# Second mixture: block products and output tiles alternate three times a pair of slices in place of eight

## The chip, the cores and the metric

The kernel runs on one core of a Trainium2 chip. The metric is the device time of one execution in microseconds (us), the median of several runs; lower is better. Five engines work side by side, each through its own list of instructions in order: TensorE (PE: matmuls; its weight loads are a row of their own, PEld), VectorE (DVE), ScalarE (ACT), GpSimd (POOL), and SyncE (SP), which issues transfers here. They wait for each other through semaphores only.

## What is computed

A gated attention over 768 steps and 16 heads gives 1536 tokens of width 384. A gated feed-forward layer (width 1536) follows, and then the second mixture: four experts of width 1024, all applied to every token and weighted. The change touches only this last part.

```python
def _moe2_ref(x, domain_probs, w1, w2) -> np.ndarray:
    N, D = x.shape                                    # 1536, 384
    E = w1.shape[0]                                   # 4
    p = domain_probs / (domain_probs.sum(-1, keepdims=True) + 1e-09)
    out = np.zeros((N, D), dtype=np.float32)
    for e in range(E):
        h = np.maximum(x @ w1[e], 0.0)                # (1536, 1024)
        out += p[:, e:e + 1] * (h @ w2[e])
    return out.astype(np.float32)
```

## The kernel before

Every matrix product is made in float32 out of three matmuls on rounded parts: high by high, high by low, low by high.

The second mixture goes through 16 pairs of slices. A pair is 256 of the 1024 hidden units of one expert. For a pair the hidden values are a 2 by 3 arrangement of blocks, two slices of 128 units by three groups of 512 tokens; each block fills one of six PSUM banks, A to F. Pair 0 is made plainly (`hidden_plain`: 54 matmuls of 512 columns in a row). Pairs 1 to 15 use a scheme with fewer multiplications: 15 **block products**, numbered 0 to 14, of sums of weight blocks with sums of token blocks. Each product is three matmuls of 512 columns (L1706 to L1708) into one bank; some banks take several products in turn. Between these, ScalarE copies a bank's state out (`keep`, L999) and VectorE adds or subtracts a kept copy to or from another bank (`combine`, L1375), so that each bank ends as a hidden block. ScalarE then applies the relu and rounds (`round_hidden`, L970: the high part), and VectorE makes the low part (`split_bank`, L1312). Only then is the bank free for the next pair.

An **output tile** is 128 tokens by 384 outputs of the previous pair's hidden values times the second weights: six matmuls of 384 columns (L1453 to L1455) into one of two small banks, out_ps0 for even tiles and out_ps1 for odd ones. There are 12 a pair, 0 to 11. VectorE adds a finished tile to the result in SBUF (`add_up`, L1329; L1326 for pair 0). TensorE may start tile n only when `add_up` of tile n - 2, which sat in the same small bank, is done (semaphore s_acc).

What sets the order is written out by hand. On TensorE it is `sums_and_outputs(pair)`: the 15 products of `pair`, with tiles of `pair - 1` between, of which the last (from `LAG` = 9 on) come in the next call, as tiles of `last - 1`. The loops over pairs on ScalarE and on VectorE are written to match. A number's place in `MULS` is its place among the products, from which the waits are worked out; `COPIES` and `ADDS` do the same for copies and combinations. For the last pair VectorE's list has an order of its own (`if pair == NPAIR - 1`). In pair 1 the rounded parts of the token sums are still being made: `split_sum` (L1318) on VectorE stands ahead of the loop, with `add_up(0, 0)` to `add_up(0, 2)` between.

After the last pair's products TensorE does what is left of pair 14's tiles and then pair 15's 12 tiles, and SyncE sends each result tile off when it is accumulated.

## Time and profile before

| | us |
|---|---|
| runs | 690.18, 690.23, 692.04 |
| median | 690.23 |
| span of the profiled execution | 689.6 |
| of it, hidden_plain and pairs 1 to 15's products and tiles, on TensorE | about 316 to 686.7 |
| one pair of slices, from a place to the same place a pair later | 23.0 |

The profiled execution's span, from its first to its last instruction, is 0.6 us under the median. No longer time of the same execution is given, so the 0.6 us stands for what lies around the span.

In the profile an engine's busy time is the sum of its instructions. TensorE's matmuls overlap each other in the records, so the distance between the starts of two matmuls tells what one costs, not its recorded length. In a timeline a row gives the start, the length, the engine, the line of the kernel, the operation, and written tile <- read tiles; a bracket at its end says how long the engine had been idle and who ended that.

### The profile page before, as it was taken

Reading aid. Unit: us, or ns where it says so; the run is one execution under the profiler, and the core shown is the slowest. Engines: PE = TensorE matmul, PEld = TensorE weight load, DVE = VectorE, ACT = ScalarE, POOL = GpSimd, SP = SyncE. Lnnn points to the kernel's source line nnn. Section 1 sums busy time; section 2 is a strip of 40 time slices with the busy share of each in tenths; the row PEclk is TensorE's granted clock in tenths of the full one; section 3 lists DMA queues with packets and bytes.
Section 4 is the critical chain, followed back from the end, with each engine's and each line's share of the span. In section 5 each row is a group of like instructions: output and inputs, shape, how many; then the busy total and the mean of one; then the engine's idle time right before and its main releaser. Section 6 shows DMA issues by size and latency. Waiting matters only on the chain.

```text
span 689.6 us, 10745 instructions
## 1 busy us (share of the span) xinstructions
PE 680.8 (99%) x3987; PEld 632.7 (92%) x3987; DVE 461.4 (67%) x820; ACT 266.4 (39%) x485; POOL 327.2 (47%) x416
## 2 busy tenths in 40 slices
PE   8999999999999999999999999999999999999998
PEld 7788999999999999998999999999999999999997
DVE  6875747555565544118978867886787678767876
ACT  4524533223522252227534333433343334343430
POOL 3569561111111116773394567456745674577200
PEclk9999999999999999999999999999999999999999
DMA  9896490009102001000011110111011101100003
GB/s 154 163 217 173 106 139 1 10 2 118 20 5 74 1 1 47 1 5 19 1 47 46 47 47 0 47 47 46 1 47 48 46 1 47 46 24 1 23 1 138
DMA packets 72230, 34.56 MB, mean 50 GB/s; under 512 B 53872, under 2 KB 71664, under 8 KB 72176
## 3 DMA queue, kind: packets, MB, share of 16 engines
q1 hardware_dynamic: 71728, 33.85, 22.8%
q8 instruction: 32, 0.52, 0.4%
q14 instruction: 22, 0.18, 0.1%
q10 hardware_dynamic: 448, 0.00, 0.0%
HBM read 30.89 MB, written 2.36 MB: 48 GB/s over the span
## 4 chain that ended last, share of the span: by engine, by line
PE 92%; SPq 3%; DVE 1%; POOL 1%; DMA 1%; issue 1%; ACT 0%; POOLq 0%
PE out_ps L1453 13%; PE out_ps L1454 13%; PE out_ps L1455 13%; PE hid_ps L1446 7%; PE hid_ps L1448 7%; PE hid_ps L1447 6%; PE at_ps L1708 5%; PE at_ps L1707 5%; PE at_ps L1706 4%; PE hid_ps L1707 2%; PE hid_ps L1708 2%; PE hid_ps L1706 2%; SPq L488 2%; PE at_ps L1531 2%; PE at_ps L1545 1%; PE at_ps L1585 1%
## 5 line engine op out<-in xcount | busy, mean ns | idle before, releaser
L1329 DVE SCALAR_TENSOR_TENSOR x<-out_ps,prob,x 128x384 f32<-128x384 f32 x180 | 110.3, 613 | 57.8 <-PE out_ps L1455 57.8
L1454 PE MATMUL out_ps<-early_r,late_r 128*128 128x384 f32 x384 | 129.4, 337 | 0.0
L1455 PE MATMUL out_ps<-early_r,late_r 128*128 128x384 f32 x384 | 129.3, 337 | 0.0
L1453 PE MATMUL out_ps<-early_r,late_r 128*128 128x384 f32 x384 | 129.0, 336 | 0.0
L722 POOL TENSOR_TENSOR hid_lo<-act_sb,hid_hi 128x384 fp32r<-128x384 f32 x44 | 44.8, 1019 | 159.6 <-ACT hid_hi L949 159.6
L999 ACT COPY late<-at_ps 128x512 f32<-128x512 f32 x105 | 61.8, 588 | 101.8 <-PE at_ps L1708 98.7
L1295 DVE TENSOR_TENSOR act_sb<-hid_ps,act_sb 128x384 f32<-128x384 f32 x48 | 26.0, 541 | 79.1 <-PE hid_ps L1448 79.1
L1453 PEld LDWEIGHTS out_ps<-early_r,late_r 128*128 128x128 f32 x384 | 72.1, 188 | 6.1 <-DVE x L1329 0.2
L1454 PEld LDWEIGHTS out_ps<-early_r,late_r 128*128 128x128 f32 x384 | 72.0, 188 | 5.6
L1455 PEld LDWEIGHTS out_ps<-early_r,late_r 128*128 128x128 f32 x384 | 72.1, 188 | 0.0
L949 ACT CAST hid_hi<-act_sb 128x384 fp32r<-128x384 f32 x48 | 24.6, 512 | 83.9 <-DVE act_sb L1295 83.9
L738 POOL TENSOR_TENSOR early<-stage 128x128 f32<-128x128 f32 x15 | 7.0, 467 | 102.4 <-PE at_ps L1708 102.4
L1708 PE MATMUL at_ps<-late_r,early_r 128*128 128x512 f32 x135 | 53.6, 397 | 0.0
L1375 DVE TENSOR_TENSOR at_ps<-at_ps,late 128x512 f32<-128x512 f32 x75 | 52.1, 695 | 0.5
L1706 PE MATMUL at_ps<-late_r,early_r 128*128 128x512 f32 x135 | 52.4, 388 | 0.0
L1446 PE MATMUL hid_ps<-xn_hi,wvh 128*128 128x384 f32 x141 | 49.2, 349 | 0.9 <-POOL wvl L652 0.9
L775 POOL TENSOR_TENSOR early_r<-early,early_r 128x1408 fp32r<-128x1408 f32 x15 | 48.5, 3236 | 0.0
L1707 PE MATMUL at_ps<-late_r,early_r 128*128 128x512 f32 x120 | 47.3, 394 | 0.0
L1448 PE MATMUL hid_ps<-xn_hi,wvl 128*128 128x384 f32 x141 | 47.3, 335 | 0.0
L1447 PE MATMUL hid_ps<-xn_lo,wvh 128*128 128x384 f32 x141 | 47.2, 335 | 0.0
L1453 PE MATMUL out_ps<-hid_hi,woh 128*128 128x384 f32 x132 | 46.3, 350 | 0.0
L1446 PE MATMUL hid_ps<-xn_hi,wgh 128*128 128x384 f32 x132 | 45.2, 342 | 0.2 <-DVE act_sb L1282 0.2
(301 smaller groups left out, 1617.4 us busy)
## 6 DMA issues: line engine op xcount, KB each, us to landing
stage<-in_moe_w_dram SPq DMA_DIRECT2D x32, 384.0 KB, 3.6
stage<-in_moe_w_out_dram SPq DMA_DIRECT2D x4, 576.0 KB, 5.4
out_dram<-x SPq DMA_DIRECT2D x12, 192.0 KB, 1.9
stage<-in_moe_w_gate_dram SPq DMA_DIRECT2D x8, 216.0 KB, 4.1
stage<-in_moe_w_val_dram SPq DMA_DIRECT2D x8, 216.0 KB, 4.2
a_tm<-in_alpha_dram SPq DMA_DIRECT2D x9, 192.0 KB, 4.5
k_tm<-in_k_dram SPq DMA_DIRECT2D x9, 192.0 KB, 5.4
q_tm<-in_q_dram SPq DMA_DIRECT2D x9, 192.0 KB, 5.3
```

Source lines behind the costliest of these rows:

```text
L999: act.copy(tcp[n], bank).then_inc(s_copy, 1)
L1329: dve.scalar_tensor_tensor(out=a, in0=part, scalar=p, in1=a, op0=ALU.mult, op1=ALU.add).then_inc(s_acc, 1)
L1375: dve.tensor_tensor(bank, bank, tcp[part], op).then_inc(s_add, 1)
L1446: pe.matmul(dst, ah, bh, start=(n == 0), stop=False)
L1447: pe.matmul(dst, ah, bl, start=False, stop=False)
L1448: mm = pe.matmul(dst, al, bh, start=False, stop=(n == last))
L1453: pe.matmul(dst, ah, bh, start=first, stop=False)
L1454: pe.matmul(dst, ah, bl, start=False, stop=False)
L1455: return pe.matmul(dst, al, bh, start=False, stop=last)
L1706: pe.matmul(bank, ah, bh, start=first, stop=False, skip_group_check=True)
L1707: pe.matmul(bank, ah, bl, start=False, stop=False, skip_group_check=True)
L1708: pe.matmul(bank, al, bh, start=False, stop=True, skip_group_check=True).then_inc(s_mul, 1)
```

## The change

TensorE's order is changed, and the two other engines' orders with it. No instruction is added or removed: the counts of products, tiles, copies and combinations stay the same.

- On TensorE a pair's products and tiles now form three groups each: products 8, 6, 10, then tiles 8 to 11 of the pair before last and tile 0 of the last; products 7, 0, 13, 12, then tiles 1 to 3; products 14, 4, 1, 11, then tiles 4 to 7; products 2, 9, 3, 5, which run on into the next pair's 8, 6, 10. `LAG` goes from 9 to 8. Products 11 and 1 change places.
- On ScalarE the copy after product 14 goes behind the rounding of bank F.
- On VectorE the `add_up` calls are spread differently. In the stretch ahead of the loop `add_up(0, 1)` and `add_up(0, 2)` are taken out from between the `split_sum` calls. The last pair no longer has an order of its own.

```diff
-        MULS = (8, 6, 10, 7, 0, 13, 12, 14, 4, 11, 1, 2, 9, 3, 5)
+        MULS = (8, 6, 10, 7, 0, 13, 12, 14, 4, 1, 11, 2, 9, 3, 5)
-        LAG = 9
+        LAG = 8
...
-                act.wait_ge(s_mul, nth(MULS, q, 14))
-                keep(4, bank_a)
                 if pair > 1:
                     act.wait_ge(s_tile, NTILE * (pair - 1))
                 act.wait_ge(s_add, nth(ADDS, q, 9))
                 round_hidden(bank_f, pair, 1, 2)
+                act.wait_ge(s_mul, nth(MULS, q, 14))
+                keep(4, bank_a)
...
             split_sum(4)
-            add_up(0, 1)
             split_sum(1)
             split_sum(2)
-            add_up(0, 2)
             split_sum(9)
...
                 combine(bank_f, 1, ALU.subtract)
-                add_up(pair - 1, 3)
+                add_up(pair - 1, 1)
                 dve.wait_ge(s_add, nth(ADDS, q, 7))
                 dve.wait_ge(s_copy, nth(COPIES, q, 2))
                 combine(bank_f, 2, ALU.subtract)
-                add_up(pair - 1, 4)
+                add_up(pair - 1, 2)
+                add_up(pair - 1, 3)
+                split_bank("F", 1, 2)
                 dve.wait_ge(s_mul, nth(MULS, q, 4))
                 dve.wait_ge(s_copy, nth(COPIES, q, 4))
                 combine(bank_d, 4, ALU.subtract)
-                split_bank("F", 1, 2)
                 dve.wait_ge(s_mul, nth(MULS, q, 11))
                 dve.wait_ge(s_copy, nth(COPIES, q, 8))
                 combine(bank_a, 8, ALU.subtract)
-                add_up(pair - 1, 5)
                 dve.wait_ge(s_mul, nth(MULS, q, 10))
                 dve.wait_ge(s_copy, nth(COPIES, q, 7))
                 combine(bank_e, 7, ALU.subtract)
+                add_up(pair - 1, 4)
+                add_up(pair - 1, 5)
+                split_bank("A", 1, 0)
                 add_up(pair - 1, 6)
-                split_bank("A", 1, 0)
                 add_up(pair - 1, 7)
...
                 split_bank("E", 0, 0)
-                add_up(pair - 1, 8)
-                split_bank("C", 0, 2)
                 dve.wait_ge(s_mul, nth(MULS, q, 5))
                 dve.wait_ge(s_copy, nth(COPIES, q, 5))
                 combine(bank_b, 6, ALU.subtract)
-                if pair == NPAIR - 1:
-                    add_up(pair - 1, 9)
+                split_bank("C", 0, 2)
                 dve.wait_ge(s_add, nth(ADDS, q, 8))
                 combine(bank_d, 5, ALU.add)
-                if pair < NPAIR - 1:
-                    add_up(pair - 1, 9)
-                add_up(pair - 1, 10)
+                add_up(pair - 1, 8)
                 dve.wait_ge(s_add, nth(ADDS, q, 1))
                 dve.wait_ge(s_copy, nth(COPIES, q, 9))
                 combine(bank_b, 9, ALU.subtract)
-                if pair == NPAIR - 1:
-                    add_up(pair - 1, 11)
+                add_up(pair - 1, 9)
                 split_bank("D", 1, 1)
-                if pair < NPAIR - 1:
-                    add_up(pair - 1, 11)
-                else:
-                    add_up(pair, 0)
+                add_up(pair - 1, 10)
                 split_bank("B", 0, 1)
-                if pair < NPAIR - 1:
-                    add_up(pair, 0)
-                add_up(pair, 1)
-                add_up(pair, 2)
-            for t in range(3, NTILE):
+                add_up(pair - 1, 11)
+                add_up(pair, 0)
+            for t in range(1, NTILE):
                 add_up(NPAIR - 1, t)
```

On TensorE the whole new order is in one place, and reads:

```diff
                 bank_free("A")
                 mul(bank_a, 8, True)
-                if q:
-                    out_tile(last - 1, 9)
-                    out_tile(last - 1, 10)
                 bank_free("F")
                 mul(bank_f, 6, True)
-                if q:
-                    out_tile(last - 1, 11)
-                out_tile(last, 0)
                 bank_free("E")
                 mul(bank_e, 10, True)
+                if q:
+                    for t in range(LAG, NTILE):
+                        out_tile(last - 1, t)
+                out_tile(last, 0)
                 kept(0)
                 mul(bank_a, 7)
                 bank_free("C")
                 mul(bank_c, 0, True)
-                out_tile(last, 1)
-                out_tile(last, 2)
                 kept(8)
                 mul(bank_f, 13)
                 bank_free("B")
                 mul(bank_b, 12, True)
-                out_tile(last, 3)
+                for t in range(1, 4):
+                    out_tile(last, t)
                 kept(2)
                 mul(bank_a, 14)
-                out_tile(last, 4)
                 bank_free("D")
                 mul(bank_d, 4, True)
+                kept(1)
+                mul(bank_b, 1)
                 kept(4)
                 mul(bank_a, 11)
-                out_tile(last, 5)
-                out_tile(last, 6)
-                kept(1)
-                mul(bank_b, 1)
-                out_tile(last, 7)
+                for t in range(4, LAG):
+                    out_tile(last, t)
                 kept(7)
                 mul(bank_d, 2)
                 kept(6)
                 mul(bank_c, 9)
                 kept(9)
                 mul(bank_e, 3)
-                out_tile(last, 8)
                 kept(3)
                 mul(bank_b, 5)
```

The order of the built programs shows it at three places. First TensorE where one pair passes into the next: products 5 (at_ps1), 8 (at_ps0) and then, before, tile 9 of the pair before last:

```order
L1706 MATMUL at_ps1<-late_r,early_r 128x512
L1707 MATMUL at_ps1<-late_r,early_r 128x512
L1708 MATMUL at_ps1<-late_r,early_r 128x512
L1706 MATMUL at_ps0<-late_r,early_r 128x512
L1707 MATMUL at_ps0<-late_r,early_r 128x512
L1708 MATMUL at_ps0<-late_r,early_r 128x512
L1453 MATMUL out_ps1<-early_r,late_r 128x384
L1454 MATMUL out_ps1<-early_r,late_r 128x384
L1455 MATMUL out_ps1<-early_r,late_r 128x384
```

TensorE at the same place after the change (its lines are numbered 11 lower): products 5, 8, then 6 (out_ps2) and 10 (hid_ps1), before any tile:

```order
L1695 MATMUL at_ps1<-late_r,early_r 128x512
L1696 MATMUL at_ps1<-late_r,early_r 128x512
L1697 MATMUL at_ps1<-late_r,early_r 128x512
L1695 MATMUL at_ps0<-late_r,early_r 128x512
L1696 MATMUL at_ps0<-late_r,early_r 128x512
L1697 MATMUL at_ps0<-late_r,early_r 128x512
L1695 MATMUL out_ps2<-late_r,early_r 128x512
L1696 MATMUL out_ps2<-late_r,early_r 128x512
L1697 MATMUL out_ps2<-late_r,early_r 128x512
L1695 MATMUL hid_ps1<-late_r,early_r 128x512
L1696 MATMUL hid_ps1<-late_r,early_r 128x512
L1697 MATMUL hid_ps1<-late_r,early_r 128x512
```

The tiles that stood between products 8, 6 and 10 now follow product 10 in one run of five.

Second, VectorE ahead of its loop and at the start of pair 1, before. L1326 is `add_up` of pair 0 (tiles 0, 1, 2, 3 in order), L1318 `split_sum`, L1312 the last block of pair 0, L1375 the first combination:

```order
L1326 TENSOR_SCALAR x2<-out_ps0,prob 128x384
L1318 TENSOR_TENSOR v_last<-early,late_r 128x512
L1312 SCALAR_TENSOR_TENSOR late_r<-hid_ps0,late_r 128x512
L1318 TENSOR_TENSOR late_r<-early,late_r 128x512
L1326 TENSOR_SCALAR x2<-out_ps1,prob 128x384
L1318 TENSOR_TENSOR late_r<-v_late,late_r 128x512
L1318 TENSOR_TENSOR late_r<-early,late_r 128x512
L1326 TENSOR_SCALAR x2<-out_ps0,prob 128x384
L1318 TENSOR_TENSOR late_r<-v_late,late_r 128x512
L1318 TENSOR_TENSOR late_r<-early,late_r 128x512 x2
L1375 TENSOR_TENSOR out_ps2<-out_ps2,late 128x512
L1326 TENSOR_SCALAR x2<-out_ps1,prob 128x384
```

VectorE at the same place after the change:

```order
L1326 TENSOR_SCALAR x2<-out_ps0,prob 128x384
L1318 TENSOR_TENSOR v_last<-early,late_r 128x512
L1312 SCALAR_TENSOR_TENSOR late_r<-hid_ps0,late_r 128x512
L1318 TENSOR_TENSOR late_r<-early,late_r 128x512
L1318 TENSOR_TENSOR late_r<-v_late,late_r 128x512
L1318 TENSOR_TENSOR late_r<-early,late_r 128x512
L1318 TENSOR_TENSOR late_r<-v_late,late_r 128x512
L1318 TENSOR_TENSOR late_r<-early,late_r 128x512 x2
L1373 TENSOR_TENSOR out_ps2<-out_ps2,late 128x512
L1326 TENSOR_SCALAR x2<-out_ps1,prob 128x384
L1373 TENSOR_TENSOR out_ps2<-out_ps2,late 128x512
L1326 TENSOR_SCALAR x2<-out_ps0,prob 128x384
```

Between `add_up` of tile 0 and of tile 1 stand eight 512-wide instructions and the first combination, where three stood.

Third, VectorE in the last pair, before, from the two combinations of bank C (at_ps2) on; L1312 are the splits of E, C, D and B, and L1329 the tiles 8, 9, 10, 11:

```order
L1375 TENSOR_TENSOR at_ps2<-at_ps2,late 128x512 x2
L1312 SCALAR_TENSOR_TENSOR late_r<-hid_ps1,late_r 128x512
L1329 SCALAR_TENSOR_TENSOR x2<-out_ps0,prob,x2 128x384
L1312 SCALAR_TENSOR_TENSOR late_r<-at_ps2,late_r 128x512
L1375 TENSOR_TENSOR at_ps1<-at_ps1,late 128x512
L1329 SCALAR_TENSOR_TENSOR x2<-out_ps1,prob,x2 128x384
L1375 TENSOR_TENSOR hid_ps0<-hid_ps0,late 128x512
L1329 SCALAR_TENSOR_TENSOR x2<-out_ps0,prob,x2 128x384
L1375 TENSOR_TENSOR at_ps1<-at_ps1,late 128x512
L1329 SCALAR_TENSOR_TENSOR x2<-out_ps1,prob,x2 128x384
L1312 SCALAR_TENSOR_TENSOR late_r<-hid_ps0,late_r 128x512
```

VectorE at the same place after the change:

```order
L1373 TENSOR_TENSOR at_ps2<-at_ps2,late 128x512 x2
L1312 SCALAR_TENSOR_TENSOR late_r<-hid_ps1,late_r 128x512
L1373 TENSOR_TENSOR at_ps1<-at_ps1,late 128x512
L1312 SCALAR_TENSOR_TENSOR late_r<-at_ps2,late_r 128x512
L1373 TENSOR_TENSOR hid_ps0<-hid_ps0,late 128x512
L1329 SCALAR_TENSOR_TENSOR x2<-out_ps0,prob,x2 128x384
L1373 TENSOR_TENSOR at_ps1<-at_ps1,late 128x512
L1329 SCALAR_TENSOR_TENSOR x2<-out_ps1,prob,x2 128x384
L1312 SCALAR_TENSOR_TENSOR late_r<-hid_ps0,late_r 128x512
L1329 SCALAR_TENSOR_TENSOR x2<-out_ps0,prob,x2 128x384
L1312 SCALAR_TENSOR_TENSOR late_r<-at_ps1,late_r 128x512
```

`add_up` of tile 8 has moved behind three more 512-wide instructions, the first of which (at_ps1) needs the copy made after product 5.

## Rows read from the trace of the kernel before

**Rows 1.** The page's chain that ended last, by engine, share of the span.

```profile
PE 92%; SPq 3%; DVE 1%; POOL 1%; DMA 1%; issue 1%; ACT 0%; POOLq 0%
```

**Rows 2.** Waits, 328 to 671 us: who waited for whom, us, times, longest.

```profile
DVE x L1329 <- PE out_ps L1455: 53.5, 69, 2.4
```

**Rows 3.** TensorE's timeline, hidden_plain: matmuls of 512 columns in one run.

```profile
318.25 0.39 PE L1455 MATMUL at_ps<-late_r,early_r 128*128 128x512 f32 x1
...
326.64 0.39 PE L1453 MATMUL hid_ps<-late_r,early_r 128*128 128x512 f32 x1
```

**Rows 4.** TensorE's timeline over one pair, 482 to 505 us.

```profile
482.24 0.39 PE L1706 MATMUL hid_ps<-late_r,early_r 128*128 128x512 f32 x1
...
491.66 0.39 PE L1706 MATMUL hid_ps<-late_r,early_r 128*128 128x512 f32 x1
...
493.74 0.33 PE L1453 MATMUL out_ps<-early_r,late_r 128*128 128x384 f32 x1
...
494.81 0.33 PE L1453 MATMUL out_ps<-early_r,late_r 128*128 128x384 f32 x1
...
495.85 0.39 PE L1706 MATMUL out_ps<-late_r,early_r 128*128 128x512 f32 x1
...
505.27 0.39 PE L1706 MATMUL hid_ps<-late_r,early_r 128*128 128x512 f32 x1
```

**Rows 5.** Timeline of all engines, 470.6 to 475.8 us.

```profile
470.71 0.33 PE L1453 MATMUL out_ps<-early_r,late_r 128*128 128x384 f32 x1
...
471.97 0.62 DVE L1329 SCALAR_TENSOR_TENSOR x<-out_ps,prob,x 128x384 f32<-128x384 f32 x1 [2.45 <-PE out_ps L1455]
...
474.20 0.33 PE L1453 MATMUL out_ps<-early_r,late_r 128*128 128x384 f32 x1
...
474.40 0.59 ACT L999 COPY late<-at_ps 128x512 f32<-128x512 f32 x1 [2.91 <-PE at_ps L1708]
...
475.09 0.70 DVE L1375 TENSOR_TENSOR out_ps<-out_ps,late 128x512 f32<-128x512 f32 x1 [1.46 <-ACT late L999]
```

**Rows 6.** TensorE's and VectorE's timelines, pair 1, 329 to 334 us.

```profile
329.36 0.33 PE L1453 MATMUL out_ps<-early_r,late_r 128*128 128x384 f32 x1
...
331.37 0.68 DVE L1318 TENSOR_TENSOR v_last<-early,late_r 128x512 fp32r<-128x512 f32 x1
...
331.97 0.68 DVE L1312 SCALAR_TENSOR_TENSOR late_r<-hid_ps,late_r 128x512 fp32r<-128x512 f32 x1
...
333.77 0.62 DVE L1326 TENSOR_SCALAR x<-out_ps,prob 128x384 f32<-128x384 f32 x1 [0.53 <-PE out_ps L1455]
```

**Rows 7.** VectorE's timeline, 671.5 to 673.7 us: two calls of add_up.

```profile
671.85 0.61 DVE L1329 SCALAR_TENSOR_TENSOR x<-out_ps,prob,x 128x384 f32<-128x384 f32 x1
...
672.97 0.61 DVE L1329 SCALAR_TENSOR_TENSOR x<-out_ps,prob,x 128x384 f32<-128x384 f32 x1
```

**Rows 8.** Weight loads (PEld) in the same stretch.

```profile
672.51 0.19 PEld L1453 LDWEIGHTS out_ps<-early_r,late_r 128*128 128x128 f32 x1 [0.21 <-DVE x L1329]
672.62 0.19 PEld L1454 LDWEIGHTS out_ps<-early_r,late_r 128*128 128x128 f32 x1
...
673.69 0.19 PEld L1453 LDWEIGHTS out_ps<-early_r,late_r 128*128 128x128 f32 x1 [0.19 <-issue]
```

**Rows 9.** Timeline of all engines, last pair's products, 665 to 670.5 us.

```profile
665.22 0.59 ACT L999 COPY late<-hid_ps 128x512 f32<-128x512 f32 x1 [0.52 <-DVE hid_ps L1375]
...
665.70 0.59 ACT L999 COPY late<-at_ps 128x512 f32<-128x512 f32 x1
...
667.66 0.40 PE L1708 MATMUL at_ps<-late_r,early_r 128*128 128x512 f32 x1
...
668.09 1.43 DVE L1375 TENSOR_TENSOR at_ps<-at_ps,late 128x512 f32<-128x512 f32 x2
...
670.35 0.33 PE L1453 MATMUL out_ps<-early_r,late_r 128*128 128x384 f32 x1
```

**Rows 10.** TensorE's timeline, its last matmul.

```profile
686.37 0.34 PE L1455 MATMUL out_ps<-early_r,late_r 128*128 128x384 f32 x1
```

## The prediction, made before the changed kernel ran

> **What bounds the kernel now.** I read the chain of work that ended last first: TensorE holds 92% of the span [rows 1], so only its time counts. Then the waits of the stretch that the change touches: from 328 to 671 us no wait of TensorE is listed. VectorE waits for finished tiles 69 times, 53.5 us in all [rows 2]; it has time to spare, but whether it has it at the right moment is another matter. Last, the distance between matmul starts, in the timelines.
>
> The reader is to see two things there. First, a matmul costs more beside a change of kind. In the long run of hidden_plain 37 distances of 512-column matmuls take 8.39 us, 0.227 each [rows 3]; deep in a tile run six 384-column matmuls take 495.85 - 494.81 = 1.04 us, 0.173 each [rows 4]. A pair lasts 505.27 - 482.24 = 23.03 us [rows 4] for 45 of the first and 72 of the second: 10.20 + 12.48 = 22.68 us bare. 0.35 us are left for eight alternations. The run of three products at 491.66 takes 2.08 us against 2.04 bare, the two tiles behind it 2.11 against 2.08 [rows 4].
>
> Second, a tile that waits for its small bank pays for more than the wait. At the end of pair 15's products, add_up ends at 671.85 + 0.61 = 672.46; the held weight load starts at 672.51, and the next load, which goes with the start of the held matmul, at 672.62 [rows 7, 8]. So from the end of add_up to the tile's first matmul 0.16 us pass. For tile 0, which has three waits, add_up ends at 673.58 and the load starts at 673.69 [rows 7, 8]: 0.11 and again 0.11, so 0.22 us. These are the prices for a bank that is freed late.
>
> **The change, part by part.** Counts stay; only places move.
>
> (a) Alternations, a gain. Eight a pair become three, all behind runs of at least 12 product matmuls. I price a run as the nine-matmul run and its tiles: 0.04 + 0.03 = 0.07 us, three make 0.21, and 0.35 - 0.21 = 0.14 us are saved a pair, 15 pairs: **-2.1 us**. Bounds: if product matmuls settle at 2.08 / 9 = 0.231 and never at 0.227, only the tile side saves, some 0.06 a pair, -0.9 us; if tiles behind a long run carry nothing, three times 0.04 remain, 0.23 saved, -3.4 us. I take the middle since pair 1 begins in the 0.227 rhythm: the run of rows 3 goes on into it.
>
> The Trainium skill, "TensorE: Matmul & The Clock Gate", Part 1, speaks against this gain: there back-to-back matmuls start N / 2.4 GHz + 2.5 ns apart whatever stands around them, 0.216 us for 512 columns; the trace shows 0.227 to 0.231. By its rule (a) is nothing, which is rival 3.
>
> (b) Tiles 3 of a pair, a wait. In the new run of tiles 1 to 3, tile 3 needs add_up(1), and VectorE does that only after the first combination, which needs the copy of bank B after product 12, the product right before the run. Today too a tile follows product 12: the run starts at 474.20, ScalarE's copy at 474.40, the combination at 475.09, 0.89 after the run's start [rows 5]. It holds VectorE 0.60 (a 512-wide instruction's distance, [rows 6]: 331.37 to 331.97), so add_up(1) starts at 1.49, ends at 2.11 (0.62, [rows 5]), and tile 3 may start at 2.27. Two tiles take 2.11. Late by 0.16 us.
>
> (c) Tile 6. Product 11 stands right before tiles 4 to 7. Its end is seen 0.20 after the run's start, as product 12's is by the copy [rows 5]; VectorE then does the combinations of A and E, 1.20, and add_up(4), 0.62: 2.02, with the price 2.18, against 2.11. Late by 0.07.
>
> (d) Tile 0 after tiles 8 to 11. A tile's add_up starts 1.26 after the tile's first matmul (470.71 to 471.97, [rows 5]). In this run a 512-wide instruction stands between every two calls, and such a step takes 672.97 - 671.85 = 1.12 us [rows 7], where a tile takes 1.04. add_up(10) therefore starts at 1.26 + 2.24 = 3.50, ends at 4.12, and tile 0 can go at 4.34; four tiles take 4.19. Late by 0.15; with tile 11, which is on the edge, 0.17.
>
> (b) to (d) make 0.40 us a pair. Nothing is behind them to absorb a loss of TensorE's own time. 14 pairs: **+5.6 us**. Before, a combination or a split also sat between calls, but products lay between the tiles and gave VectorE the time back. Bound from below: if the freed bank is seen in 0.05 (the held load alone) and 0.11 for tile 0, without the 0.11 behind it, (b), (c) and (d) are 0.05, 0 and 0.06: +1.5 us. From above: each restart also brings back the uneven rhythm behind a switch, 0.03: +1.3 more.
>
> (e) Pair 1, a wait of its own. Tile 0 now follows product 10: 329.36 + three matmuls of 0.227 = 330.04 instead of 329.36 [rows 6]. add_up(0) starts 1.26 later, 331.30, holds 0.53, then come eight 512-wide instructions, 4.80, to 336.63, the combination, 0.60, and add_up(1), 0.62, to 337.85; tile 3 can go at 338.01. TensorE is there at 330.04 + 1.07 (tile 0) + 2.76 (twelve product matmuls) + 2.11 (two tiles) = 335.98. Today tile 1's add_up ran at 333.77, inside the splits [rows 6]. **+2.0 us**.
>
> (f) Last pair. Tiles 8 and on follow product 5 with no products of a next pair between. From the last matmul of product 9 (667.66, [rows 9]): VectorE's two combinations of bank C end at 668.09 + 1.43, that is 1.86; ScalarE rounds C at 1.90 and can begin the copy after product 5 0.48 later (665.22 to 665.70, [rows 9]), which ends at 2.97; the combination of B starts at 3.02 and, with the split of C and the combination of D, holds VectorE 1.80; add_up(8) ends at 5.44, and tile 10 can go at 5.60. TensorE is there after seven matmuls and two tiles, 1.59 + 2.11 = 3.70. 1.9 us late, and the next three tiles lose 0.08 each by the 1.12 step: 2.15. What this place costs today goes off: 15 tiles in a row from 670.35 [rows 9] to 686.37 [rows 10] take 16.02 us for 89 distances of 0.173, 15.43, so 0.5 beside the switch. **+1.7 us**.
>
> ScalarE's moved copy after product 14 has one answer: product 11 needs it only after products 4 and 1, 1.4 us, and the rounding ahead of it takes 0.6. DMAs and GpSimd keep their order; both work a pair ahead. What follows the last matmul is as now.
>
> **Sum.** -2.1 + 5.6 + 2.0 + 1.7 = +7.2 us: span 689.6 + 7.2 = 696.8, and on the median, 0.6 above the span, 690.23 + 7.2, I say **697.4 us**, 1.0% slower.
>
> **Rivals.**
>
> 1. The pairs' own waits don't come: add_up is done before the bank is wanted. It is decided at 0.07 to 0.17 us of lateness. For it: TensorE slowed by (e) gives VectorE some room, and small delays may shift. Against: VectorE's chain in (b) starts at TensorE's own product 12 in every pair, so a delay moves both. Then -2.1 + 2.0 + 1.7 = +1.6: 691.8, not slower by more than a measurement tells. That a difference of 0.3%, 2.1 us, is about what this measurement can tell from none is used throughout. If (e) and (f) don't come either, the change does only (a): 688.1, just faster.
>
> 2. A late bank costs only the held load's delay. Then +1.5 in the pairs and 0.1 less in (e) and (f) each: -2.1 + 1.5 + 3.5 = +2.9, 693.1. Against it: the next load stands 0.11 behind the held one [rows 8].
>
> 3. The alternations cost nothing, as the page's rule has it, and all the waits come: +9.3, 699.5. Against it: the 0.35 us that a pair has over the bare distances.
>
> 4. Restarts bring the uneven rhythm back, or a fourth tile of each pair is late too (tile 10 and tile 2 have under 0.1 us left by the sums above): 3 x 0.03 and 0.05 a pair, +2: 699.4 to 700.5.
>
> **How the numbers follow.** Forecast 0.60 (695.5 to 698.8); rival 1 with the pairs' waits gone 0.09, with all gone 0.03; rival 2 0.12; rival 3 0.06; rival 4 0.10. The range is to leave out no more than 0.2: from rival 2's 693.1, which is the bound of the waits' price, to 699.5, the end of (a)'s. It leaves out rival 1, and half of rival 4. Faster by over 0.3%: 0.03. Within 0.3%: 0.09. Slower: 0.88.
>
> **What would show it.** In the changed kernel's waits, weight loads at the tile lines should be held by VectorE's L1329, three times a pair. A pair should last 23.03 - 0.14 + 0.40 = 23.29 us. In pair 1 TensorE should stand still for some 2 us near 336 us, and again near the end, ahead of pair 14's tile 10. Product matmuls late in a run of 21 should stand 0.227 apart. VectorE's first combination should follow product 12's tile run by 0.89. The prediction is wrong if the pair's length is 22.9 (rival 1), if the two long stops are missing, or if the distances in long runs stay at 0.231.

## The result, and the profile after

| | before | changed |
|---|---|---|
| median, us | 690.45 | 698.62 |
| runs, us | 690.18, 690.23, 690.68, 692.04 | 697.76, 697.86, 699.39, 699.72 |
| spans of the changed kernel's runs, us | | 696.0, 696.1, 697.6, 698.0 |

The ratio is 1.0114, 95% interval 1.0102 to 1.0125: slower by 1.1%. The forecast was 697.4, 693.1 to 699.5.

The page of the changed kernel, its engines' busy times and its chain that ended last (cf. [rows 1]):

```profile
PE 684.6 (98%) x3987; PEld 629.8 (90%) x3987; DVE 462.4 (66%) x820; ACT 262.2 (38%) x485; POOL 327.8 (47%) x416
PE 94%; DVE 4%; issue 1%; ACT 1%; DMA 0%; SPq 0%; ACTq 0%; DVEq 0%
```

VectorE, 1% of the chain before, holds 4% now, though it is idle for a third of the span. The waits of 328 to 680 us say where (cf. [rows 2]; who waited for whom, us, times, longest):

```profile
DVE out_ps L1373 <- ACT late L999: 39.6, 14, 2.8
DVE x L1329 <- PE out_ps L1444: 18.9, 56, 0.4
...
PEld out_ps L1442 <- DVE x L1329: 4.9, 15, 2.0
...
PEld out_ps L1442 <- issue: 2.6, 14, 0.2
PEld out_ps L1442 <- DVE x L1326: 2.2, 1, 2.2
PE out_ps L1442 <- DVE x L1326: 1.8, 1, 1.8
PE out_ps L1442 <- DVE x L1329: 1.7, 1, 1.7
```

Before, TensorE had no listed wait from 328 to 671 us, and two loads of 0.2 us each behind that. Now its weight loads are held by `add_up`: two long ones (2.2 us in pair 1, 2.0 in the last) and two short ones of 0.2 us in each of 14 pairs (tile 3: 14 of the 15 under L1329; tile 0: the 14 under "issue"). A third, at tile 6, is too short to be listed. VectorE's waits for a finished tile shrink from 53.5 to 18.9 us, but its spare time is not gone: its waits for ScalarE's copies ahead of the combinations grow from 20.5 us to 49.0 (39.6 in the first row, 9.4 for other banks). It idles at another place.

The whole stage, TensorE's first product and its last matmul:

```profile
326.77 0.39 PE L1695 MATMUL at_ps<-late_r,early_r 128*128 128x512 f32 x1
...
692.70 0.34 PE L1444 MATMUL out_ps<-early_r,late_r 128*128 128x384 f32 x1
```

That is 365.93 us. Before, the first product starts at 328.00 and the last matmul at 686.37 [rows 10]: 358.37. This stretch is called the stage below. It is **7.55 us** longer, against 7.2 forecast. The spans differ by only 6.4 since the part ahead of the stage, which the change doesn't touch, was 1.2 us shorter in this profile. I compare kernels by this stage below.

TensorE's timeline over one pair, from the start of product 2 to the next pair's product 2 (cf. [rows 4], 23.03 us):

```profile
484.75 0.39 PE L1695 MATMUL hid_ps<-late_r,early_r 128*128 128x512 f32 x1
...
489.56 0.33 PE L1442 MATMUL out_ps<-early_r,late_r 128*128 128x384 f32 x1
...
494.95 0.39 PE L1695 MATMUL at_ps<-late_r,early_r 128*128 128x512 f32 x1
...
508.04 0.39 PE L1695 MATMUL hid_ps<-late_r,early_r 128*128 128x512 f32 x1
```

508.04 - 484.75 = 23.29 us. The rows show the run of 21 product matmuls (4.81) and the five tiles behind it (5.39 for 30 x 0.1733 = 5.20). Weight loads at tile 3 of such a pair (cf. [rows 8]):

```profile
499.47 0.19 PEld L1444 LDWEIGHTS out_ps<-early_r,late_r 128*128 128x128 f32 x1
499.87 0.19 PEld L1442 LDWEIGHTS out_ps<-early_r,late_r 128*128 128x128 f32 x1 [0.21 <-DVE x L1329]
499.98 0.19 PEld L1443 LDWEIGHTS out_ps<-early_r,late_r 128*128 128x128 f32 x1
```

The held load is at 499.87 and the next 0.11 behind it; the two together set tile 3 back by 0.16 us. What holds it starts, as forecast, 0.89 us behind the first tile after product 12:

```profile
404.51 0.33 PE L1442 MATMUL out_ps<-early_r,late_r 128*128 128x384 f32 x1
...
405.40 0.70 DVE L1373 TENSOR_TENSOR out_ps<-out_ps,late 128x512 f32<-128x512 f32 x1 [2.83 <-ACT late L999]
```

The stop of pair 1 (cf. [rows 6]), on TensorE and, in the second block, on VectorE:

```profile
334.57 0.34 PE L1444 MATMUL out_ps<-early_r,late_r 128*128 128x384 f32 x1
336.76 0.45 PE L1442 MATMUL out_ps<-early_r,late_r 128*128 128x384 f32 x1 [1.85 <-DVE x L1326]
```

```profile
330.15 0.62 DVE L1326 TENSOR_SCALAR x<-out_ps,prob 128x384 f32<-128x384 f32 x1 [0.43 <-PE out_ps L1444]
...
336.10 0.60 DVE L1326 TENSOR_SCALAR x<-out_ps,prob 128x384 f32<-128x384 f32 x1
```

`add_up(1)` comes 5.95 us after `add_up(0)`, ends at 336.70, and tile 3 starts at 336.76: 2.19 us after the last matmul instead of 0.17, and 0.11 more behind it. The same in the last pair (cf. [rows 9]), TensorE:

```profile
675.87 0.34 PE L1444 MATMUL out_ps<-early_r,late_r 128*128 128x384 f32 x1
677.87 0.44 PE L1442 MATMUL out_ps<-early_r,late_r 128*128 128x384 f32 x1 [1.66 <-DVE x L1329]
```

### The profile page after: what moved, and what is told of

It is laid out like the page before. It is cut to its first block, busy times and chain, and to the rows that moved or that the text cites. A ratio compares the mean times of both kernels' runs of the same rounds, so it can differ in the third digit from the quotient of the medians.

```text
span 696.0 us, 10745 instructions
## 1 busy us (share of the span) xinstructions
PE 684.6 (98%) x3987; PEld 629.8 (90%) x3987; DVE 462.4 (66%) x820; ACT 262.2 (38%) x485; POOL 327.8 (47%) x416
## 4 chain that ended last, share of the span: by engine, by line
PE 94%; DVE 4%; issue 1%; ACT 1%; DMA 0%; SPq 0%; ACTq 0%; DVEq 0%
PE out_ps L1442 14%; PE out_ps L1444 13%; PE out_ps L1443 13%; PE hid_ps L1435 7%; PE hid_ps L1437 7%; PE hid_ps L1436 7%; PE at_ps L1696 4%; PE at_ps L1697 4%; PE at_ps L1695 4%; PE hid_ps L1696 2%; PE hid_ps L1697 2%; PE at_ps L1520 2%; PE hid_ps L1695 2%; PE at_ps L1534 2%; PE at_ps L1574 1%; PE at_ps L1544 1%
## 5 line engine op out<-in xcount | busy, mean ns | idle before, releaser
L1329 DVE SCALAR_TENSOR_TENSOR x<-out_ps,prob,x 128x384 f32<-128x384 f32 x180 | 110.1, 612 | 24.0 <-PE out_ps L1444 24.0
L999 ACT COPY late<-at_ps 128x512 f32<-128x512 f32 x105 | 60.3, 590 | 70.0 <-PE at_ps L1697 68.3
L970 ACT ACTIVATE late_r<-hid_ps 128x512 fp32r<-128x512 f32 x32 | 19.1, 598 | 83.7 <-PE hid_ps L1697 59.2
L1373 DVE TENSOR_TENSOR out_ps<-out_ps,late 128x512 f32<-128x512 f32 x30 | 20.8, 694 | 39.6 <-ACT late L999 39.6
```

The source lines that it names most:

```text
L999: act.copy(tcp[n], bank).then_inc(s_copy, 1)
L1329: dve.scalar_tensor_tensor(out=a, in0=part, scalar=p, in1=a, op0=ALU.mult, op1=ALU.add).then_inc(s_acc, 1)
L1373: dve.tensor_tensor(bank, bank, tcp[part], op).then_inc(s_add, 1)
```

## The experiments

Ten kernels; e10 is the changed one once more. "Stage" is from TensorE's first product to its last matmul in the profile, against the 358.37 us of before; "pair" is the mean length of 13 pairs in that profile; "clock" is the mean granted clock of the profiled run.

| | ratio (95%) | stage | pair, us | clock |
|---|---|---|---|---|
| changed | 1.0114 (1.0102 to 1.0125) | +7.55 | 23.30 | 1.000 |
| e1_steady | 1.0046 (1.0032 to 1.0059) | +4.65 | 22.99 | 0.997 |
| e2_pair1 | 1.0077 (1.0061 to 1.0092) | +5.47 | 23.31 | 1.000 |
| e3_last | 1.0094 (1.0079 to 1.0110) | +5.99 | 23.31 | 0.999 |
| e4_all | 0.9986 (0.9977 to 0.9995) | -0.78 | 22.98 | 1.000 |
| e5_dose | 1.0268 (1.0251 to 1.0285) | +19.60 | 24.05 | 0.998 |
| e6_copy4 | 1.0219 (1.0202 to 1.0236) | +14.91 | 23.79 | 1.000 |
| e7_addup12 | 1.0099 (1.0082 to 1.0116) | +7.14 | 23.31 | 1.000 |
| e8_stop | 1.0097 (1.0080 to 1.0114) | +6.36 | 22.97 | 0.998 |
| e9_order | 0.9993 (0.9983 to 1.0002) | -0.91 | 22.97 | 1.000 |
| e10_changed | 1.0124 (1.0107 to 1.0140) | +9.12 | 23.31 | 0.998 |

### e1_steady: the three late calls of each pair

```diff
+                if pair > PLAIN:
+                    add_up(pair - 1, 1)
                 dve.wait_ge(s_mul, nth(MULS, q, 13))
                 dve.wait_ge(s_copy, nth(COPIES, q, 1))
                 combine(bank_f, 1, ALU.subtract)
...
                 combine(bank_a, 8, ALU.subtract)
+                add_up(pair - 1, 4)
...
                 combine(bank_e, 7, ALU.subtract)
-                add_up(pair - 1, 4)
...
                 add_up(pair - 1, 9)
-                split_bank("D", 1, 1)
                 add_up(pair - 1, 10)
-                split_bank("B", 0, 1)
+                split_bank("D", 1, 1)
                 add_up(pair - 1, 11)
+                split_bank("B", 0, 1)
```

> The changed kernel with three edits to VectorE's order alone, in the pairs after pair 1: add_up(1) ahead of the first combination, add_up(4) ahead of the combination of E with copy 7, add_up(10) ahead of the split of D. TensorE's and ScalarE's orders stay as changed. Theory (late add_up calls are the price, (b) to (d) of the prediction): the changed kernel's trace has 0.39 us of lateness a pair at tiles 3, 6, 11 and 0, so 14 x 0.39 = 5.5 us go: 7.6 - 5.5 = 2.1 us above the kernel before, a pair of 23.29 - 0.39 = 22.90 us; the two long stops of 2.0 us (pair 1 and last pair) stay. Rival A (the loss lies in TensorE's new order or in ScalarE's moved copy and rounding, which this leaves alone): no change, 7.6 above, 23.29 a pair. Rival S (VectorE is simply behind, a wait taken away here comes back at the next tile): a pair of 23.2 or more, at most 1.5 us gained. If the alternations were worth nothing, (a) = 0, the pair would be 23.03 and the kernel 4.0 us above the kernel before.

The pair falls from 23.30 to 22.99 us and none of TensorE's waits between 346 and 670 us is left. Rivals A and S are out: VectorE's order alone took the time. But the pair was to be 22.90; of 0.39 us of lateness, 0.31 came back (see e4 and e9). The stage is 2.9 us shorter than the changed kernel's, 4.5 when 1.6 us are left out that the profile of this run shows and the forecast did not have: behind the stop of pair 1 TensorE's granted clock fell (see e10).

### e2_pair1 and e3_last: the two stops

e2 gives pair 1 nearly the order of before on the three engines, in branches `if q == 0:` (products 1 and 11 keep their new order, with tiles 5 to 7 together behind them), and puts `add_up(0, 1)` and `add_up(0, 2)` back among the splits. e3 is, for the last pair:

```diff
                 if pair == NPAIR - 1:
+                    split_bank("E", 0, 0)
+                    add_up(pair - 1, 8)
+                    split_bank("C", 0, 2)
+                    dve.wait_ge(s_mul, nth(MULS, q, 5))
+                    dve.wait_ge(s_copy, nth(COPIES, q, 5))
+                    combine(bank_b, 6, ALU.subtract)
+                    add_up(pair - 1, 9)
...
                 if pair == NPAIR - 1:
+                    out_tile(last, LAG)
                 kept(3)
                 mul(bank_b, 5)
```

> The changed kernel with pair 1 alone back in the order of the kernel before, on TensorE, VectorE and ScalarE; all later pairs as changed. Theory: step (e) goes, 2.1 us by the changed kernel's trace, and nothing comes in its place: 7.6 - 2.1 = 5.5 us above the kernel before, no stop of TensorE near 336 us, and the pairs behind it still 23.29 us. Rival S (the first hidden pair has a backlog of VectorE's from the eight splits, whichever order stands there): under 0.5 us gained, the stop shifts to a later tile of pair 1 or of pair 2. Rival A': part of the 0.39 a pair behind it is carried over from pair 1's lateness, then the pairs get shorter as well and more than 3 us go.

> The changed kernel with the last pair alone edited: tile 8 of the pair before goes ahead of product 5 again, and VectorE takes add_up(8) to add_up(11) and the last split in an order near that of the kernel before. Theory: of step (f)'s 1.7 us nearly all goes, 1.6: 6.0 us above the kernel before; the stop of 1.9 us ahead of pair 14's tile 10 shrinks to under 0.3. Rival: the stop comes from ScalarE's chain (round C, copy 5, combination of B), which the last pair needs in any order; then it only moves to another tile and under 0.5 us is gained.

e2's stage is 2.09 us shorter than the changed kernel's, e3's 1.57: step (e) goes whole, (f) but for 0.1 of its 1.7, and no new stop takes their place. The pairs behind pair 1 stay at 23.31, so their lateness isn't inherited from pair 1.

### e4_all: what remains of the alternations

> The three edits above in one kernel: TensorE's three alternations a pair from pair 2 on, with VectorE's add_up calls early enough, pair 1 as before, and the last pair's tile 8 ahead of product 5. Theory: only (a) is left, 14 pairs x -0.14 = -2.0 us, and 0.1 to 0.2 us at the last pair: 1.8 us under the kernel before, 688.4 us, ratio 0.9974, a pair of 22.89 us against 23.03. Rival 3 of the prediction (alternations cost nothing): 690.4, pair 23.03. If the effects of the three edits do not add up (waits that move on): 690 to 693.

With the waits gone the kernel beats the one before, 689.89 against 691.02 us; by the ratio it is 1.0 us, by the stage 0.8, where 1.8 was expected. One pair of it:

```profile
388.97 0.39 PE L1744 MATMUL hid_ps<-late_r,early_r 128*128 128x512 f32 x1
...
411.96 0.39 PE L1744 MATMUL hid_ps<-late_r,early_r 128*128 128x512 f32 x1
```

22.99 us; the mean is 22.98, 0.06 under before, where 0.14 was forecast. The missing 0.08 lies in the tile runs. The run behind 21 product matmuls takes 5.25 to 5.29 us for 5.20 bare, the one of four tiles 4.21 to 4.25 for 4.16. VectorE and the weight loads in one of them:

```profile
373.19 0.61 DVE L1333 SCALAR_TENSOR_TENSOR x<-out_ps,prob,x 128x384 f32<-128x384 f32 x1
```

```profile
373.60 0.19 PEld L1493 LDWEIGHTS out_ps<-early_r,late_r 128*128 128x128 f32 x1
373.85 0.19 PEld L1491 LDWEIGHTS out_ps<-early_r,late_r 128*128 128x128 f32 x1
373.96 0.19 PEld L1492 LDWEIGHTS out_ps<-early_r,late_r 128*128 128x128 f32 x1
```

`add_up(9)` ends at 373.80, the load of tile 11 starts 0.05 later, 0.25 behind the one ahead of it where 0.17 to 0.18 is regular. No wait is listed, and still the load is 0.08 late: a near miss. In each run of more than two tiles the third tile comes as close: `add_up` of two tiles before ends 0.23 us ahead of the third tile's first matmul, whose load regularly starts 0.17 ahead.

### e5_dose: a dose of lateness

```diff
                 combine(bank_f, 1, ALU.subtract)
-                add_up(pair - 1, 1)
+                if pair == PLAIN:
+                    add_up(pair - 1, 1)
                 dve.wait_ge(s_add, nth(ADDS, q, 7))
                 dve.wait_ge(s_copy, nth(COPIES, q, 2))
                 combine(bank_f, 2, ALU.subtract)
+                if pair > PLAIN:
+                    add_up(pair - 1, 1)
```

> The changed kernel with one edit to VectorE's order: from pair 2 on, add_up(1) goes one step later, behind the second combination of bank F, so that the suspected cost is made larger. Theory (the lateness of add_up is paid one for one, since nothing behind it gives time back): tile 3 is late by 0.16 + at least the 0.60 of one more 512-wide instruction in each of 14 pairs, 0.75 to 0.90 in all: a pair of 23.9 to 24.0 us, 8.4 to 10.3 us over the changed kernel. Rival (VectorE's lateness is partly made up by the products behind the tiles, so only a share of it reaches TensorE): less than 5 us. The stops are 0.8 us long; if stops of this length made TensorE's clock fall as the 1.9 us stop of the first experiment's profile did near 337 us (granted 0.87 in 330 to 340), it would be seen in each pair and cost several us more.

Waits of this kernel, 346 to 690 us:

```profile
PEld out_ps L1445 <- DVE x L1329: 13.2, 14, 0.9
```

VectorE in one pair, the two combinations in one row and `add_up(1)` and `add_up(2)` in the next:

```profile
409.17 1.44 DVE L1373 TENSOR_TENSOR out_ps<-out_ps,late 128x512 f32<-128x512 f32 x2 [2.83 <-ACT late L999]
...
410.51 1.13 DVE L1329 SCALAR_TENSOR_TENSOR x<-out_ps,prob,x 128x384 f32<-128x384 f32 x2
```

`add_up(1)` starts 1.34 us after the first combination where it was 0.60 (406.00 - 405.40 in the changed kernel): 0.74 later. The pair grows by 0.75: the lateness is paid one for one. In 14 pairs that is 10.5 us, and the rest of the +12.05 on the changed kernel is the clock's fall in pair 1 (1.57). The 0.8 us stops do nothing to the clock, which is granted at 1.00 over all of 346 to 690 us.

### e6_copy4: ScalarE's moved copy

```diff
                 act.wait_ge(s_add, nth(ADDS, q, 9))
+                act.wait_ge(s_mul, nth(MULS, q, 14))
+                keep(4, bank_a)
                 round_hidden(bank_f, pair, 1, 2)
-                act.wait_ge(s_mul, nth(MULS, q, 14))
-                keep(4, bank_a)
```

> The changed kernel with only ScalarE's order undone: the copy after product 14 (copy 4) stands ahead of the rounding of bank F again. It tells whether the moved copy, to which the prediction gave no cost and no gain, does anything. Theory (one order, all three engines): the changed kernel has add_up calls 1, 2 and 3 and the split of F close together, so the rounding of F would now come one copy, 0.48 to 0.60 us, later, VectorE's split of F and all behind it with it, and tile 6 is late by that much more: 14 x 0.5 = +7 us over the changed kernel. Rival (ScalarE has time to spare, 262 busy of 696 us, the place of one copy costs nothing): no change within 1 us.

Waits of this kernel, 328 to 690 us:

```profile
PEld out_ps L1442 <- DVE x L1329: 13.2, 29, 2.0
```

Stage +7.36 on the changed kernel, and the held loads double (29 where 15 were): the new one is at tile 6, whose lateness goes from 0.07 to 0.55 by the distances of its matmuls. So the size came as expected, 0.5 a pair, but not by the way that the expectation gives. In one pair of this kernel:

```profile
406.83 0.70 DVE L1373 TENSOR_TENSOR out_ps<-out_ps,late 128x512 f32<-128x512 f32 x1 [2.83 <-ACT late L999]
...
410.16 0.59 ACT L999 COPY late<-at_ps 128x512 f32<-128x512 f32 x1 [3.43 <-PE at_ps L1697]
410.64 0.61 ACT L970 ACTIVATE late_r<-out_ps 128x512 fp32r<-128x512 f32 x1
411.28 0.69 DVE L1312 SCALAR_TENSOR_TENSOR late_r<-out_ps,late_r 128x512 fp32r<-128x512 f32 x1 [1.20 <-ACT late_r L970]
```

and the rounding of F in the changed kernel:

```profile
407.31 0.60 ACT L970 ACTIVATE late_r<-out_ps 128x512 fp32r<-128x512 f32 x1 [2.02 <-DVE out_ps L1373]
```

Copy 4 waits for product 14, behind the tile run, and holds the rounding of F with it: the rounding starts 3.81 us after the first combination (410.64 - 406.83) where it was 1.91 (407.31 - 405.40). That is 1.9 us later, not one copy; VectorE then waits 1.20 us for it, and its slack takes up all but 0.5. That the size came out as expected is luck. An engine that is idle 62% of the span makes the kernel 1% slower by the order of two of its instructions. The prediction was right to charge the move nothing, but didn't see that VectorE's new order depends on it.

### e7_addup12: moving the call instead of the work

```diff
             split_sum(2)
+            add_up(0, 1)
             split_sum(9)
             split_sum(3)
+            add_up(0, 2)
             split_sum(5)
```

(and the same two calls dropped in pair 1.)

> The changed kernel with VectorE's add_up(1) and add_up(2) of the very first tiles back among the eight splits ahead of pair 1; TensorE and ScalarE as changed. The prediction's step (e) said that the stop in pair 1 is add_up(1) behind eight splits. Naive theory: it goes with this edit, 2.1 us gained on the changed kernel, as when all of pair 1 was put back (1.6 us gained by the traces' stage). Rival S (VectorE has 8 splits plus the combinations to do before pair 1's product 11, whichever way; the stop moves to a product matmul that waits for ScalarE's copy 4 near 340 us): a stop of some 1.5 us there, 0.5 us gained at most. I hold S for likelier, since add_up's two places only swap with 512-wide instructions that TensorE's product run needs too.

Waits of 328 to 345 us:

```profile
PE at_ps L1699 <- ACT late L999: 1.3, 1, 1.3
```

By the stage 0.41 us are gained, and the tile's stop is gone (e2 gained 2.09 by the stage; the 1.6 in the expectation is the difference of the two profiles' spans). TensorE now stands at a product matmul that needs ScalarE's copy. Together with e2 this shows that step (e)'s place was right while its cause is wider: the stop isn't tied to the call's place. That TensorE's product run in pair 1 comes earlier than the eight splits plus the combinations can be done fits both runs, but is argued. Only e2, which puts all three engines' orders back in pair 1, removed the stop; no run tells which of the three it takes.

### e8_stop and e10_changed: TensorE's clock behind a stop

e10 is the changed kernel unaltered. e8 is e1 with, in pair 1 only, `add_up(1)` behind the second combination and the split of F.

```diff
                 combine(bank_f, 2, ALU.subtract)
+                if pair == PLAIN:
+                    split_bank("F", 1, 2)
+                    add_up(pair - 1, 1)
                 add_up(pair - 1, 2)
                 add_up(pair - 1, 3)
```

> The changed kernel once more, unaltered, for the spread of its runs and TensorE's granted clock in them. Theory (its stop of 2.0 us in pair 1 lets the clock fall in part of the runs): runs in two groups, the upper with a mean clock of 0.997 to 0.998 and spans near 697.7, the lower with 1.000 and spans near 696.1; if the profiled run is of the upper group, its trace shows the fall right behind the stop near 337 us. Rival (the spread comes from the part ahead of the first product, which differs by up to 1.2 us between profiles): spans in no relation to the clock.

> The kernel of the first experiment (add_up calls early in the pairs) with the stop of pair 1 made longer: add_up(1) there goes behind the second combination of F and the split of F, 1.2 to 2.1 us later. It measures TensorE's clock after a stop. In the first experiment the profile fell to a granted clock of 0.87 in 330 to 340 us and 0.96 in 340 to 350, and its runs stood in two groups (spans 691.3, 691.8 and 693.3 three times); the changed kernel's own runs do as well (696.0, 696.1 and 697.6, 698.0). Theory (the fall comes from the stop, and a stop of 2.0 us is near the point where it happens or not): a stop of 3.2 to 4.1 us brings the fall in every run, all spans in one group, 693.3 plus the longer stop: 694.5 to 695.5, with a granted clock under 0.9 near 340 us. Rival (the two groups are something else, such as DMA placement): two groups 1.7 to 2 us apart again, and a profile that need not show a fall.

The stretches around the stop, of e10 (stretch, us; busy; granted clock; DMA):

```profile
334.00:338.00 4.00, 2.15 (x12) 0.96 0.01 2
338.00:342.00 4.00, 4.00 (x14) 0.61 0.00 0
342.00:346.00 4.00, 4.00 (x24) 1.00 0.02 6
```

and of the changed kernel's first profile, with the same stop, 1.85 us idle:

```profile
338.00:342.00 4.00, 4.00 (x21) 1.00 0.02 4
```

14 matmuls in place of 21. TensorE's timeline of e10 there:

```profile
337.30 0.44 PE L1442 MATMUL out_ps<-early_r,late_r 128*128 128x384 f32 x1 [1.85 <-DVE x L1326]
...
338.12 0.52 PE L1442 MATMUL out_ps<-early_r,late_r 128*128 128x384 f32 x1
338.44 0.52 PE L1443 MATMUL out_ps<-early_r,late_r 128*128 128x384 f32 x1
...
339.51 0.63 PE L1696 MATMUL at_ps<-v_last,early_r 128*128 128x512 f32 x1
339.94 0.63 PE L1697 MATMUL at_ps<-late_r,early_r 128*128 128x512 f32 x1
...
341.17 0.40 PE L1697 MATMUL hid_ps<-late_r,early_r 128*128 128x512 f32 x1
```

From 337.80, half a microsecond after the restart, to 341.17 a matmul costs 0.32 us (384 columns) and 0.43 (512): the lower of the clock's two levels, 1.2 GHz, for 3.4 us. e10's stage is 9.12 - 7.55 = **1.57 us** longer than that of the first profile, with the same stop, and 1.53 of it lie in these two runs of matmuls. e1 shows the fall too; its runs stand at 691.3 and 691.8 (mean clock 1.000) and at 693.3, 693.3 and 693.4 (0.997). In e10 two of four runs have 0.998 (698.1, 698.7). With the longer stop of e8 (4.28 us between matmul starts) all four runs have 0.995 to 0.998:

```profile
340.00:344.00 4.00, 4.00 (x12) 0.57 0.02 4
```

In the kernels without the stop of pair 1 (e2, e4, e9) 25 of 26 runs have a mean of 1.000 and one 0.999. e3, e5 and e6, which have the stop too, have 0.998 in one, two and one of four runs. So the theory holds: the stop sometimes costs 1.6 us on top of itself. But the clock is not the only thing that spreads the runs. e8's spans are not one group (694.9, 695.0, 695.7, 696.6), the two upper ones with 0.995; and a run of e10 and one of the first four stand at 697.5 and 697.6 with 1.000. The 11 spans of e9, which has no stop in pair 1, run from 687.7 to 689.6, and the two longest have a clock of 1.000. The part ahead of the stage differs by 0.7 us among the eleven profiles of the changed orders (first product at 326.77 to 327.47; 328.00 before), which is not enough for the 1.5 us between 696.1 and 697.6. The cause of this second spread is open. The stop near the end, 1.66 us idle, lowered the clock in no profile.

### e9_order: the near misses

```diff
                 split_bank("E", 0, 0)
+                split_bank("C", 0, 2)
...
                 combine(bank_b, 6, ALU.subtract)
-                split_bank("C", 0, 2)
                 dve.wait_ge(s_add, nth(ADDS, q, 8))
                 combine(bank_d, 5, ALU.add)
-                add_up(pair - 1, 8)
                 dve.wait_ge(s_add, nth(ADDS, q, 1))
                 dve.wait_ge(s_copy, nth(COPIES, q, 9))
                 combine(bank_b, 9, ALU.subtract)
+                add_up(pair - 1, 8)
                 add_up(pair - 1, 9)
```

> The kernel with all three edits (the one whose pair took 22.96 us), with one more change of VectorE's order from pair 2 on: the split of C goes ahead of the combination of B with copy 6, where VectorE waits 0.62 us for ScalarE, and the combination of B with copy 9 ahead of add_up(8), so that no 512-wide instruction stands between add_up(8), add_up(9) and add_up(10). In that kernel's long tile run tile 11's weight load is 0.1 us behind its place, and the uneven rhythm (0.185, 0.176, 0.182 in place of 0.173) appears behind such near misses. Theory (near misses cost 0.03 to 0.06 a pair): the run of 30 matmuls falls from 5.26 to 5.29 us to 5.23 to 5.25, a pair from 22.96 to 22.92, 0.4 to 0.6 us less in all: 689.3 us, 1.5 us under the kernel before. Rival (the rhythm is set by the switch alone): no difference of either beyond 0.1 us.

The long run shrinks, but only from a mean of 5.27 us to 5.26 (5.24 to 5.29), and the pair's mean stays at 22.97, where e4's is 22.98 (not 22.96). The stage gains 0.13 us, a quarter of what the theory gave. By time e9 can't be told from e4, and not from the kernel before either: its interval, 0.9983 to 1.0002, includes 1. The edit removes the near miss at tile 11; the third tile of every run is as close to an `add_up` as in e4. So the 512-wide instruction between two calls is not what costs most of the 0.08 us a pair. It may be the length of a tile's own circle (its matmuls, `add_up`, the next load), which the third tile of a run meets without slack; no run here tells.

## Why the prediction was right

- **The sum.** +7.2 forecast, +7.55 in the stage. The terms as measured, -1.7 (14 x -0.12) + 5.5 + 2.1 + 1.7, make 7.6: each came, and no large errors cancel.
- **(a)** In the changed kernel the pair takes 23.30 with 0.39 of lateness in it, 22.91 without: -0.12 against the forecast -0.14. The product runs are as priced: 21 matmuls in 4.80 us, settling at 0.227 after nine. But the term isn't one that can be kept apart: in e1, e4 and e9, with the banks in time, only -0.04 to -0.06 is left. What came back there are near misses as in e4, which no term of the prediction held. For a kernel without waits rival 3, alternations at no price, is a little nearer than the forecast, though e4 is faster than the kernel before (0.8 us by the stage; its interval leaves out 1, e9's does not).
- **(b), (c), (d)** Measured from the matmul distances of the changed kernel: tile 3 0.16 late (forecast 0.16), tile 6 0.07 (0.07), tiles 11 and 0 0.16 (0.17). The price of a late bank, 0.16 and 0.22, held, and rival 2 is out. Rival 1 is out by e1 and e5: the lateness is paid one for one. Rival 4 is out by the pair, 23.30 for 23.29 forecast: behind a held load the distances of the next matmuls are 0.175, 0.174, 0.175, 0.173 in most pairs, so a restart seldom brings back the uneven rhythm. One sign came in another form: of the three held loads a pair only tile 3's is listed under L1329; tile 0's stands under "issue", and tile 6's in no list.
- **(e)** 2.12 us for 2.0, at 336.8 us. The arithmetic held; that the stop would go away with `add_up(1)` in its old place (e7) was not claimed, and would have been wrong.
- **(f)** +1.7 for +1.7: the last tile run is 2.3 us over 0.1733 a matmul (18.77 for 95 distances) where it was 0.6 (16.02 for 89), with the stop of 1.9 us in front of pair 14's tile 10. e3 got 1.57 back.
- **ScalarE's copy.** The move was priced at nothing, and no loss by it shows in the terms above. But the reason given looked at product 11 alone; e6 shows that the old place would have cost 7.4 us, by the rounding of F that waits behind the copy.
- **The median** is 1.2 us above the forecast, 698.6 for 697.4. 0.35 is the sum's, and 0.2 the median of before, 690.45 in place of 690.23. TensorE's clock behind the stop of pair 1, 1.57 us in some of the runs, is a term that isn't in the prediction, but it explains the median only in part: of the two upper runs 699.72 has a clock of 0.998 and 699.39, on which the median rests, 1.000. What makes that run long is not shown.
- **Wrong without consequence:** that 0.6 us lie around the span. In every run with both figures it is 1.7 to 1.9 (697.76 for a span of 696.0); so the profiled execution of before, with its span of 689.6, took some 691.3 and was one of the longer ones. Since the sum went onto the median, this cancelled.

## What to carry to other kernels

Where one engine bounds and another hands it buffers back, an order is priced by the instant at which each buffer comes free, not by busy shares: VectorE was idle a third of the time and ScalarE 62%, and the places of one to four of their instructions a pair were worth 4 to 10 us (e1, e5, e6). Longer runs of one kind save the switches (0.06 us a pair here, 0.8 in all) but use up the slack between buffer and user; with the two small banks here the third tile of a run had none left. Before a stop is dissolved by moving the call that it waits for, look whether the work around it fits at all (e7). And an expectation that comes true in its size can still have the path wrong (e6): look at the instruction that is said to be late.

## What was not expected of the hardware

- A stop of TensorE of 1.85 us idle is followed in some executions by 3.4 us at the lower clock, 1.57 us lost (e10); the same stop in another execution of the same kernel by nothing (the first profile). The Trainium skill, "TensorE: Matmul & The Clock Gate", Part 1, gives N / 1.2 GHz between starts at the lower level, 0.427 us for 512 columns; the trace agrees (339.94 - 339.51 = 0.43).
- A weight load that is only 0.08 us late (e4, 373.85) is listed with no wait, and the matmuls there stand 0.176 and 0.195 apart in place of 0.173; the waits' view alone would call such a kernel free of them.
- The distances behind a switch to products repeat within 2 ns in nearly all such runs of all the profiles (0.229, 0.233, 0.236, 0.224, 0.231, 0.236, 0.228, 0.233, 0.231, then 0.227): a run's length can be read off before it is built.
